# A mixed attention and feed-forward kernel: products nobody reads taken out of round 0, a copy split over two engines, keys and row moves issued in another order

## The chip, the cores and the metric

One core of a Trainium2 chip runs the whole program. The metric is device time in microseconds (us), the median of three runs. TensorE (PE in the profile) multiplies, VectorE (DVE), ScalarE (ACT) and GpSimd (POOL) do the elementwise work, and SyncE (SP) only issues DMAs; ACT issues a few DMAs too. "PEld" is the loading of a matmul's stationary operand.

## The reference, cut to what matters

```python
for t in range(S):                      # attention: B=4, H=8, S=768, D=48
    cur = einsum('bhd,bhe->bhde', u * k_t, v_t)
    y_t = einsum('bhd,bhde->bhe', r_t, state + cur)
    state = w_t[..., None] * state + einsum('bhd,bhe->bhde', k_t, v_t)
x = y as (B*S, H*D)                     # 3072 tokens x 384
x = ((x @ w_a) * (x @ w_b)) @ w_out     # "gated": 1536 wide
h = x @ w_in                            # "leaky": 2048 wide
out = (max(h, 0) + alpha * min(h, 0)) @ w_out2
```

## The kernel before, in words

The attention is worked in eight rounds ("duos", n = 0 to 7). A round takes four pairs of heads over half a sequence, in two streams j = 0 and 1, and has eleven phases. Phase 0 multiplies the leaf blocks (`leaf`). Phases 2 to 6 are the levels 1 to 5 (`level`): a level multiplies keys by queries, stream 0 first and then stream 1, 96 TensorE instructions in all; then DVE scales the keys of stream 0 (`step_k`, L889), merges the first half of the products into `a_sb` (`merge_level`, L905), scales the keys of stream 1 and merges the second half, while the queries are scaled by `step_r` (in round 0 on POOL, L464). The next level's stream j needs the scaled keys and queries of stream j. The last level is not merged but copied into `a_sb` by ACT (`copy_last_level`, four copies of 32 x 384). Phase 7 turns the keys (`turn_keys`, L691), phases 8 and 9 form key-value products (`key_values`, L705) from which DVE carries the states (`carry_states`, L926, one chain a stream), then come `weighted_values` (L719) and in phase 10 `outputs` (L732). ACT copies the outputs out of PSUM (`copy_outputs`), DVE subtracts to get their low parts (`lower_outputs`, L962), and six small DMAs (`move_rows`, L336) move the rows of the last unit from `f_y` into `x_parts`.

The outputs of round n are tile n of the gated layer. Its twelve blocks (`up_a`, `up_b`, `down`, L163 to L165: three products of high and low parts) form the loop over g; one phase of the next round stands between two blocks. Before that loop, steps 0 to 11 (round 0 and the leaf of round 1) run with nothing between them but `keep_clock`: five products of 128 x 384 into `acc[0]` after each of the steps 2 to 8, ten after step 10, and three smaller ones (`keep_clock_early`) about the leaf. Nobody reads them; `acc[0]` is started anew by the first `down`. Before `up_a(0)`, TensorE waits for the copied and lowered outputs and for all six moves (`moved`).

Weights come in pieces of two blocks. SP loads piece p into one of three stages (`load_piece`, six DMAs for a piece of w_a or w_b, one for w_out), ACT splits off the high part (`split_hi`, L135), POOL for the pieces 0 to 5 and DVE after that the low part (`split_lo`, L140), which frees the stage for piece p + 3. `HI_AT` and `LO_AT` give the steps at which ACT and POOL split the pieces 0 to 5; at the steps of `LO_AT` SP also issues the load of piece p + 3. Each engine's queue is in program order, so SP at step 9 stands ahead of SP at step 10, where the moves and then the loads of the next decays (`load_w`) are.

The keys of the next round are scaled by u into `k_scratch` (`prepare_k`) before that round's leaf. In round 0 ACT does this for round 1 at the end of step 10, behind the copying of the outputs and the two moves that it issues itself.

Of the kernel before, what the change touches and what calls it, by code (L numbers as in the profile page):

```python
# [35 lines left out]
HI_AT = [2, 3, 4, 11, 11, 11]  # L36
LO_AT = [7, 8, 9, 11, 11, 11]
X_LOAD, X_SPLIT = 4, 8
OUTPUTS, MOVES = 6, 6
CLOCK_PRODUCTS = 10  # L40
# [145 lines left out]
def copies(duo, what, j, side):  # L186

    return (6 + OUTPUTS) * duo + (0 if what == "level" else 2 + 2 * j) + side + 1


def outputs_copied(duo, part):

    return (6 + OUTPUTS) * duo + 6 + part + 1
# [43 lines left out]
def front(nc, ctx, r, k, w, v, constants, y, alpha, out, shared):  # L237

    with ExitStack() as room, ExitStack() as names:
# [30 lines left out]
        with ExitStack() as room:  # L270
# [17 lines left out]
            products_done, merged, copied = sems("products_done"), sem("merged"), sem("copied")  # L288
            states_done, lowered, moved = sems("states_done"), sem("lowered"), sem("moved")
# [56 lines left out]
            def _(sp):  # L346
# [36 lines left out]
                def move_last_unit(n):  # L383

                    sp.wait_ge(copied, outputs_copied(n, OUTPUTS - 1))
                    sp.wait_ge(lowered, outputs_lowered(n, OUTPUTS - 1))
                    for q in range(KT if n > 0 else 2):
                        for row0 in (0, 64):
                            move_rows(sp, n, q, row0)
# [106 lines left out]
            def _(act):  # L496
# [29 lines left out]
                def copy_last_level(n, hd):  # L526

                    for j in range(2):
                        act.wait_ge(products_done[j], after(n, 5))
                    act.wait_ge(merged, merges(n, 4, 1))  # L530
                    for row0 in (0, 64):
                        done = copy(view(a_sb, S * hd + 32, [[BLOCK, 2 * CH], [1, 32]], 32, row0),
                                    view(products, level_bank(5, hd), [[32, 2 * CH], [1, 32]], 32, row0))
                    done.then_inc(copied, 1)
# [15 lines left out]
                def attend(step):  # L550
                    n, phase = divmod(step, PHASES)
                    if phase == 6:
                        copy_last_level(n, 0)
                    elif phase == 7:
                        copy_kt(n, 0)
                        copy_kt(n, 1)
                    elif phase == 10:
                        copy_outputs(n)
                        if n == 0:
                            act.wait_ge(lowered, OUTPUTS)  # L560
                            for row0 in (0, 64):
                                move_rows(act, n, 2, row0)

                def attend_late(step):
                    n, phase = divmod(step, PHASES)
                    if phase == 6:
                        copy_last_level(n, 1)
                    elif phase == 7 and n + 1 < DUOS:
                        prepare_r(n + 1, 0)
                        if n == 0:  # L570
                            prepare_r(n + 1, 1)
                    elif phase == 8 and 0 < n and n + 1 < DUOS:
                        prepare_k(n + 1, 0)
                        prepare_r(n + 1, 1)
                    elif phase == 9 and 0 < n and n + 1 < DUOS:
                        prepare_k(n + 1, 1)
                    elif phase == 10 and n == 0:
                        prepare_k(n + 1, 0)
                        prepare_k(n + 1, 1)
# [60 lines left out]
            def _(pe):  # L640
# [40 lines left out]
                def turn_keys(n, j):  # L681

                    if j == 0:
                        pe.wait_ge(merged, merges(n, 4, 1))
                    else:
                        pe.wait_ge(copied, copies(n, "level", 0, 1))
# [23 lines left out]
                def weighted_values(n, j):  # L710

                    pe.wait_ge(merged, merges(n, 4, 1))
                    pe.wait_ge(copied, copies(n, "level", 0, 1))
# [103 lines left out]
                def keep_clock(count):  # L817

                    pe.wait_ge(shared.w_hi_ready, 1)
                    w_hi, _ = shared.parts("w_a", 0, 0)  # L820
                    x, _ = shared.parts("w_a", 0, 0, TT)
                    for _ in range(count):
                        pe.matmul(acc[0][:, 0:TT], w_hi, x, start=True, stop=True)  # L823

                def keep_clock_early():

                    pe.matmul(acc[0][:, 0:BANK // 2], k_scratch[0][0:D, 0:P], k_scratch[0][0:D, 0:BANK // 2], start=True, stop=True)

                pe.wait_ge(products_cleared, 1)
                leaf(0, 0)  # L830
                keep_clock_early()
                keep_clock_early()
                leaf(0, 1)
                keep_clock_early()
                for step in range(1, BEFORE_TILES):
                    attend(step)
                    if 2 <= step <= 8:
                        keep_clock(CLOCK_PRODUCTS // 2)
                    elif step == PHASES - 1:
                        keep_clock(CLOCK_PRODUCTS)  # L840
# [18 lines left out]
            def _(dve):  # L859
# [39 lines left out]
                def merge_level(n, hd, phase):  # L899
# [7 lines left out]
                                        view(products, level_bank(phase, hd), [[32, 2 * CH], [h, 32 // h], [1, h]], P)).then_inc(merged, 1)  # L907

# [62 lines left out]
                def attend(step):  # L971
# [20 lines left out]
                    elif phase == 6 and n > 0:  # L992
                        last_step_k(n, 1)
# [288 lines left out]
```

## Time and profile before

| | |
|---|---|
| median of 3 runs | 1037.98 us (1037.82 to 1039.22) |
| the profiled execution's own time | 1041.41 us |
| its span, first to last instruction | 1039.5 us |
| mean granted clock | 0.997 |
| TensorE busy | 1016.9 us (98%) |
| DVE, ACT, POOL busy | 553.0, 295.7, 33.2 us |

All times of rows count from the start of the span. In a row of the timeline, "x96" means 96 instructions merged; the time is that of the whole group, and square brackets give the idle time ahead of it with what ended it. The granted clock is in parts of full speed: 1.00 is 2.4 GHz, 0.50 is 1.2 GHz.

### The profile page before, as it was taken

What the parts mean: (1) busy time and instruction counts of PE and PEld (TensorE: products, weight loads), DVE (VectorE), ACT (ScalarE), POOL (GpSimd) and SP (SyncE); (2) the same over time, 40 slices, a digit from 0 to 9 for tenths busy, and PEclk for the clock granted to TensorE, in tenths of its full rate; (3) what the DMA queues carried; (4) which work ended last, traced back from release to release, by engine and by line L of the source; (5) the groups of instructions that cost most, each with busy time, mean ns of one, the idle gap of its engine ahead of it and who ended that gap; (6) DMA issues with size and microseconds to landing.
All of it is one profiled execution on the core that took longest, in us unless ns stands there. A gap on an engine that the chain in (4) does not pass through costs nothing.

```text
span 1039.5 us, 29138 instructions
## 1 busy us (share of the span) xinstructions
PE 1016.9 (98%) x12499; PEld 988.2 (95%) x12499; DVE 553.0 (53%) x1154; ACT 295.7 (28%) x620; POOL 33.2 (3%) x29
## 2 busy tenths in 40 slices
PE   6879999999999999999999999999999999999998
PEld 5779989999999999999999999999999999999998
DVE  6357664574655645646532345645554555455454
ACT  3243513324224133142222333322222222222211
POOL 3420020000000000000000000000000000000000
PEclk9989999999999999999999999999999999999999
DMA  7244241211301312111011232110101010101000
GB/s 181 75 102 129 75 135 30 58 56 29 90 25 34 84 52 62 29 52 37 3 32 51 72 97 81 42 46 1 46 2 46 1 45 0 45 0 46 1 24 23
DMA packets 42168, 53.03 MB, mean 51 GB/s; under 512 B 5184, under 2 KB 42048, under 8 KB 42048
## 3 DMA queue, kind: packets, MB, share of 16 engines
q1 hardware_dynamic: 40624, 51.04, 17.1%
q8 instruction: 95, 1.56, 0.6%
q10 hardware_dynamic: 1424, 0.23, 0.2%
q14 instruction: 25, 0.20, 0.1%
HBM read 39.46 MB, written 9.44 MB: 47 GB/s over the span
## 4 chain that ended last, share of the span: by engine, by line
PE 94%; DVE 2%; issue 1%; DMA 1%; ACT 1%; SPq 0%; POOL 0%; ACTq 0%; DVEq 0%
PE products L163 17%; PE products L164 16%; PE products L165 16%; PE acc L163 11%; PE acc L165 11%; PE acc L164 11%; PE products L677 6%; PE products L691 1%; PE acc L823 1%; PE products L719 1%; PE products L705 1%; PE products L732 1%; PE products L654 1%; DVE f_y L877 1%; DMA w_v<-in_w_dram 1%
## 5 line engine op out<-in xcount | busy, mean ns | idle before, releaser
L163 PE MATMUL products<-x_parts,weights_hi 128*128 128x384 f32 x576 | 201.8, 350 | 0.9
L164 PE MATMUL products<-x_parts,weights_hi 128*128 128x384 f32 x576 | 195.0, 339 | 0.0
L165 PE MATMUL products<-x_parts,weights_lo 128*128 128x384 f32 x576 | 194.6, 338 | 0.0
L1169 DVE TENSOR_SCALAR leaky_low<-products,leaky_al 128x384 f32<-128x384 f32 x128 | 79.1, 618 | 169.4 <-PE products L165 169.3
L1029 DVE TENSOR_TENSOR g_sb<-a_g,products 128x384 f32<-128x384 f32 x96 | 53.2, 554 | 202.2 <-issue 118.7
L1116 ACT ACTIVATE leaky_g_hi<-leaky_g_sb 128x384 fp32r<-128x384 f32 x128 | 67.3, 525 | 295.0 <-DVE leaky_g_sb L1174 295.0
L498 ACT ACTIVATE g_hi<-g_sb 128x384 fp32r<-128x384 f32 x96 | 50.3, 524 | 244.5 <-DVE g_sb L1029 244.5
L163 PEld LDWEIGHTS products<-x_parts,weights_hi 128*128 128x128 f32 x576 | 108.7, 189 | 5.0 <-issue 1.6
L165 PEld LDWEIGHTS products<-x_parts,weights_lo 128*128 128x128 f32 x576 | 108.9, 189 | 0.0
L164 PEld LDWEIGHTS products<-x_parts,weights_hi 128*128 128x128 f32 x576 | 108.9, 189 | 0.0
L163 PE MATMUL acc<-g_hi,weights_hi 128*128 128x384 f32 x288 | 97.7, 339 | 2.4 <-DVE g_lo L1035 1.8
L165 PE MATMUL acc<-g_hi,weights_lo 128*128 128x384 f32 x288 | 97.5, 338 | 0.0
L164 PE MATMUL acc<-g_lo,weights_hi 128*128 128x384 f32 x288 | 96.9, 336 | 0.0
L498 ACT ACTIVATE a_g<-products 128x384 f32<-128x384 f32 x96 | 47.3, 493 | 132.0 <-PE products L165 132.0
L1035 DVE TENSOR_TENSOR g_lo<-g_sb,g_hi 128x384 fp32r<-128x384 f32 x96 | 53.5, 557 | 38.2 <-ACT g_hi L498 38.0
L1156 DVE TENSOR_TENSOR leaky_g_lo<-leaky_g_sb,leaky_g_hi 128x384 fp32r<-128x384 f32 x128 | 70.4, 550 | 5.2 <-ACT leaky_g_hi L1116 4.7
L677 PEld LDWEIGHTS products<-r_in,k_in 48*64 48x64 f32 (+1 forms) x3840 | 60.7, 139 | 12.4 <-issue 10.5
L1174 DVE SCALAR_TENSOR_TENSOR leaky_g_sb<-products,leaky_low 128x384 f32<-128x384 f32 x128 | 70.6, 552 | 0.3
L677 PE MATMUL products<-r_in,k_in 48*64 48x32 f32 (+1 forms) x3840 | 65.4, 223 | 1.0 <-POOL r_in L464 0.7
L164 PE MATMUL products<-x_parts,leaky_rest_hi 128*128 128x384 f32 x192 | 65.0, 339 | 0.0
L163 PE MATMUL products<-x_parts,leaky_rest_hi 128*128 128x384 f32 x192 | 64.9, 338 | 0.0
L165 PE MATMUL products<-x_parts,leaky_rest_lo 128*128 128x384 f32 x192 | 64.9, 338 | 0.0
(86 smaller groups left out, 1789.4 us busy)
## 6 DMA issues: line engine op xcount, KB each, us to landing
k_in<-in_k_dram SPq DMA_DIRECT2D x16, 336.0 KB, 4.0
r_in<-in_r_dram SPq DMA_DIRECT2D x16, 336.0 KB, 5.2
stage<-in_w_out_dram SPq DMA_DIRECT2D x14, 384.0 KB, 3.2
w_v<-in_v_dram SPq DMA_DIRECT2D x16, 288.0 KB, 3.3
y_dram<-x_in SPq DMA_DIRECT2D x8, 576.0 KB, 3.2
x_in<-y_dram SPq DMA_DIRECT2D x8, 576.0 KB, 4.5
out_dram<-leaky_out_sb SPq DMA_DIRECT2D x7, 576.0 KB, 3.3
stage<-in_w_dram SPq DMA_DIRECT2D x10, 336.0 KB, 4.0
```

Source lines behind the costliest of these rows:

```text
L163: pe.matmul(out, w_hi, x_hi, start=first, stop=False)
L164: pe.matmul(out, w_hi, x_lo, start=False, stop=False)
L165: return pe.matmul(out, w_lo, x_hi, start=False, stop=last)
L498: return act.activation(out, in_, ACT.Copy)
L654: last = pe.matmul(view(products, stream_bank(j, hd) + BLOCK * c, [[1, BLOCK]], BLOCK, BLOCK * par), key_blocks(k_scratch[j], hd, c, par), ...
L677: last = pe.matmul(view(products, level_bank(phase, hd) + 32 * (CH * j + c), [[1, 32]], rows, BLOCK * par), key_blocks(k_in[j], hd, c, par ...
L1029: dve.tensor_tensor(g_sb[:, :], a_g[:, :], b_ps(g), ALU.mult).then_inc(g_ready, 1)
L1035: dve.tensor_tensor(g_lo[f % 2][:, :], g_sb[:, :], g_hi[f % 2][:, :].bitcast(F32), ALU.subtract).then_inc(g_lo_ready, 1)
L1116: return act.activation(out_, in_, ACT.Copy)
L1156: dve.tensor_tensor(self.g_lo[f % 4][:, :], self.g_sb[f % 2][:, :], self.g_hi[f % 4][:, :].bitcast(F32), ALU.subtract).then_inc(self.g_lo_ ...
L1169: dve.tensor_scalar(self.low[f % 2][:, :], h, 0.0, self.al[:, f:f + 1], ALU.min, ALU.mult).then_inc(self.low_ready, 1)
L1174: dve.scalar_tensor_tensor(self.g_sb[f % 2][:, :], h, 0.0, self.low[f % 2][:, :], ALU.max, ALU.add).then_inc(self.g_ready, 1)
```

## The change

It has five parts. (1) All of `keep_clock` and `keep_clock_early` goes, 48 calls. (2) Of the last level's four copies, DVE takes two; ACT's two wait for the merge of their own half only, and `turn_keys` and `weighted_values` wait for both engines. (3) In round 0, ACT prepares the keys of round 1 at step 9, ahead of the outputs. (4) Piece 3 is split at step 9 and not at step 11, high and low part; with it SP loads piece 6 at step 9, ahead of the moves. (5) The moves go block by block: SP moves block 2 as soon as the outputs' parts 0 to 3 are there, and then the others; in round 0, SP moves the blocks 2 and 0 and ACT block 1 (before: SP 0 and 1, ACT 2).

```diff
--- before.py
+++ after.py
@@ -33,11 +33,10 @@
 DUOS, PHASES = UNITS // 2, 11
 F_AT = {2: 0, 4: S // 2, 8: S // 2 + S // 4, 16: S - S // 8, 32: S - S // 16, 64: S - S // 32}
 BEFORE_TILES = PHASES + 1
-HI_AT = [2, 3, 4, 11, 11, 11]
-LO_AT = [7, 8, 9, 11, 11, 11]
+HI_AT = [2, 3, 4, 9, 11, 11]
+LO_AT = [7, 8, 9, 9, 11, 11]
 X_LOAD, X_SPLIT = 4, 8
 OUTPUTS, MOVES = 6, 6
-CLOCK_PRODUCTS = 10
 STAGES = 3
 STAGED_FROM = 3
 
@@ -185,12 +184,12 @@
 
 def copies(duo, what, j, side):
 
-    return (6 + OUTPUTS) * duo + (0 if what == "level" else 2 + 2 * j) + side + 1
+    return (5 + OUTPUTS) * duo + (0 if what == "level" else 1 + 2 * j) + side + 1
 
 
 def outputs_copied(duo, part):
 
-    return (6 + OUTPUTS) * duo + 6 + part + 1
+    return (5 + OUTPUTS) * duo + 5 + part + 1
 
 
 def outputs_lowered(duo, part):
@@ -286,6 +285,7 @@
             f_done, r_stepped = sem("f_done"), sems("r_stepped")
             k_first, k_stepped, k_last = sems("k_first"), sems("k_stepped"), sems("k_last")
             products_done, merged, copied = sems("products_done"), sem("merged"), sem("copied")
+            last_level_copied = sem("last_level_copied")
             states_done, lowered, moved = sems("states_done"), sem("lowered"), sem("moved")
             a_done, b_done, a_copied, g_ready = sem("a_done"), sem("b_done"), sem("a_copied"), sem("g_ready")
             g_hi_ready, g_lo_ready, down_done, x2_copied = sem("g_hi_ready"), sem("g_lo_ready"), sem("down_done"), sem("x2_copied")
@@ -382,9 +382,10 @@
 
                 def move_last_unit(n):
 
-                    sp.wait_ge(copied, outputs_copied(n, OUTPUTS - 1))
-                    sp.wait_ge(lowered, outputs_lowered(n, OUTPUTS - 1))
-                    for q in range(KT if n > 0 else 2):
+                    for q in ((2, 0, 1) if n > 0 else (2, 0)):
+                        part = 3 if q == 2 else OUTPUTS - 1
+                        sp.wait_ge(copied, outputs_copied(n, part))
+                        sp.wait_ge(lowered, outputs_lowered(n, part))
                         for row0 in (0, 64):
                             move_rows(sp, n, q, row0)
 
@@ -523,14 +524,14 @@
                     copy(every_other(r_leaf[j], 1), every_other(queries_of(n, j), 1))
                     scaled(r_leaf[j], queries_of(n, j), 0, j).then_inc(r_prepared[j], 1)
 
-                def copy_last_level(n, hd):
+                def copy_last_level(n):
 
                     for j in range(2):
                         act.wait_ge(products_done[j], after(n, 5))
-                    act.wait_ge(merged, merges(n, 4, 1))
+                    act.wait_ge(merged, merges(n, 4, 0))
                     for row0 in (0, 64):
-                        done = copy(view(a_sb, S * hd + 32, [[BLOCK, 2 * CH], [1, 32]], 32, row0),
-                                    view(products, level_bank(5, hd), [[32, 2 * CH], [1, 32]], 32, row0))
+                        done = copy(view(a_sb, 32, [[BLOCK, 2 * CH], [1, 32]], 32, row0),
+                                    view(products, level_bank(5, 0), [[32, 2 * CH], [1, 32]], 32, row0))
                     done.then_inc(copied, 1)
 
                 def copy_kt(n, j):
@@ -550,7 +551,7 @@
                 def attend(step):
                     n, phase = divmod(step, PHASES)
                     if phase == 6:
-                        copy_last_level(n, 0)
+                        copy_last_level(n)
                     elif phase == 7:
                         copy_kt(n, 0)
                         copy_kt(n, 1)
@@ -559,13 +560,11 @@
                         if n == 0:
                             act.wait_ge(lowered, OUTPUTS)
                             for row0 in (0, 64):
-                                move_rows(act, n, 2, row0)
+                                move_rows(act, n, 1, row0)
 
                 def attend_late(step):
                     n, phase = divmod(step, PHASES)
-                    if phase == 6:
-                        copy_last_level(n, 1)
-                    elif phase == 7 and n + 1 < DUOS:
+                    if phase == 7 and n + 1 < DUOS:
                         prepare_r(n + 1, 0)
                         if n == 0:
                             prepare_r(n + 1, 1)
@@ -574,7 +573,7 @@
                         prepare_r(n + 1, 1)
                     elif phase == 9 and 0 < n and n + 1 < DUOS:
                         prepare_k(n + 1, 1)
-                    elif phase == 10 and n == 0:
+                    elif phase == 9 and n == 0:
                         prepare_k(n + 1, 0)
                         prepare_k(n + 1, 1)
 
@@ -683,7 +682,8 @@
                     if j == 0:
                         pe.wait_ge(merged, merges(n, 4, 1))
                     else:
-                        pe.wait_ge(copied, copies(n, "level", 0, 1))
+                        pe.wait_ge(copied, copies(n, "level", 0, 0))
+                        pe.wait_ge(last_level_copied, n + 1)
                     pe.wait_ge(k_last[j], n + 1)
                     for c in range(CH):
                         for hd in range(2):
@@ -710,7 +710,8 @@
                 def weighted_values(n, j):
 
                     pe.wait_ge(merged, merges(n, 4, 1))
-                    pe.wait_ge(copied, copies(n, "level", 0, 1))
+                    pe.wait_ge(copied, copies(n, "level", 0, 0))
+                    pe.wait_ge(last_level_copied, n + 1)
                     pe.wait_ge(states_done[j], states_after(n))
                     for c in range(CH):
                         for par in range(2):
@@ -814,30 +815,9 @@
                                                  f == 0, f == F1 - 1)
                     product.then_inc(down_done, 1)
 
-                def keep_clock(count):
-
-                    pe.wait_ge(shared.w_hi_ready, 1)
-                    w_hi, _ = shared.parts("w_a", 0, 0)
-                    x, _ = shared.parts("w_a", 0, 0, TT)
-                    for _ in range(count):
-                        pe.matmul(acc[0][:, 0:TT], w_hi, x, start=True, stop=True)
-
-                def keep_clock_early():
-
-                    pe.matmul(acc[0][:, 0:BANK // 2], k_scratch[0][0:D, 0:P], k_scratch[0][0:D, 0:BANK // 2], start=True, stop=True)
-
                 pe.wait_ge(products_cleared, 1)
-                leaf(0, 0)
-                keep_clock_early()
-                keep_clock_early()
-                leaf(0, 1)
-                keep_clock_early()
-                for step in range(1, BEFORE_TILES):
+                for step in range(BEFORE_TILES):
                     attend(step)
-                    if 2 <= step <= 8:
-                        keep_clock(CLOCK_PRODUCTS // 2)
-                    elif step == PHASES - 1:
-                        keep_clock(CLOCK_PRODUCTS)
                 for g in range(TILES * F1):
                     up_a(g)
                     if slot_at(g - 1):
@@ -905,6 +885,16 @@
                     dve.copy_predicated(view(a_sb, S * hd + h, [[BLOCK, 2 * CH], [2 * h, 32 // h], [1, h]], P),
                                         view(level_mask, 32 * (phase - 1), [[0, 2 * CH], [h, 32 // h], [1, h]], P).bitcast(I32),
                                         view(products, level_bank(phase, hd), [[32, 2 * CH], [h, 32 // h], [1, h]], P)).then_inc(merged, 1)
+
+                def copy_last_level(n):
+
+                    for j in range(2):
+                        dve.wait_ge(products_done[j], after(n, 5))
+                    dve.wait_ge(merged, merges(n, 4, 1))
+                    for row0 in (0, 64):
+                        done = dve.tensor_copy(view(a_sb, S + 32, [[BLOCK, 2 * CH], [1, 32]], 32, row0),
+                                               view(products, level_bank(5, 1), [[32, 2 * CH], [1, 32]], 32, row0))
+                    done.then_inc(last_level_copied, 1)
 
                 def carry_states(n, j):
 
@@ -989,8 +979,10 @@
                         if n > 0:
                             step_r(n, 0, phase - 1)
                             step_r(n, 1, phase - 1)
-                    elif phase == 6 and n > 0:
-                        last_step_k(n, 1)
+                    elif phase == 6:
+                        if n > 0:
+                            last_step_k(n, 1)
+                        copy_last_level(n)
                     elif phase == 7 and n > 0:
                         step_r(n, 0, 5)
                         step_r(n, 1, 5)
```

## Rows read from the trace of the kernel before

**Rows 1.** Waits of TensorE over the span: us in total, times, longest.

```profile
PE products L654 <- ACT k_scratch L503: 3.8, 1, 3.8
...
PE acc L163 <- DVE g_lo L1035: 1.8, 1, 1.8
```

**Rows 2.** Timeline of TensorE up to the first tile: start, us, what.

```profile
14.22 2.79 PE L677 MATMUL products<-r_in,k_in 48*64 48x32 f32 x96 [0.29 <-DVE a_sb L895]
...
26.16 1.97 PE L823 MATMUL acc<-weights_hi 128*128 128x384 f32 x5
...
32.67 1.51 PE L677 MATMUL products<-r_in,k_in 48*32 48x32 f32 x96
...
36.00 2.81 PE L691 MATMUL products<-ident,k_in 48*64 48x48 f32 x96
...
40.64 1.21 PE L705 MATMUL products<-w_v,k_scratch 64*48 64x48 f32 x48
...
43.68 0.83 PE L705 MATMUL products<-w_v,k_scratch 64*48 64x48 f32 x48
...
51.12 0.32 PE L732 MATMUL products<-r_in,state 48*48 48x64 f32 x4 [2.06 <-issue]
51.36 2.03 PE L823 MATMUL acc<-weights_hi 128*128 128x384 f32 x10
57.16 2.71 PE L654 MATMUL products<-r_leaf,k_scratch 48*64 48x64 f32 x96 [3.77 <-ACT k_scratch L503]
59.80 0.69 PE L163 MATMUL products<-x_parts,weights_hi 128*128 128x384 f32 x1
```

**Rows 3.** Windows of TensorE: busy, granted clock (PEclk), DMA share, GB/s.

```profile
26.20:28.10 1.90, 1.90 (x13) 1.00 0.00 0
...
59.80:64.10 4.30, 4.30 (x17) 0.50 0.47 132
64.10:70.00 5.90, 5.90 (x35) 0.98 0.58 160
```

**Rows 4.** Timeline of VectorE: level 3, the carried states, the first g_sb.

```profile
26.30 0.58 DVE L905 COPY_PREDICATED a_sb<-level_mask,products 128x384 f32<-128x384 int32 x1 [0.62 <-PE products L677]
26.78 0.94 DVE L889 TENSOR_TENSOR k_in<-k_in,f_y 112x384 f32<-112x384 f32 x1
...
42.22 1.97 DVE L926 SCALAR_TENSOR_TENSOR state<-state,f_y,products 112x48 f32<-112x48 f32 x10
...
65.38 0.56 DVE L1029 TENSOR_TENSOR g_sb<-a_g,products 128x384 f32<-128x384 f32 x1 [4.39 <-issue]
```

**Rows 5.** Timeline of GpSimd, level 3 and the pieces 0 to 2.

```profile
25.15 2.15 POOL L464 TENSOR_TENSOR r_in<-r_in,f_y 112x384 f32<-112x384 f32 x2 [2.42 <-PE products L677]
...
36.92 5.40 POOL L140 TENSOR_TENSOR weights_lo<-stage,weights_hi 128x768 fp32r<-128x768 f32 x3
```

**Rows 6.** Timeline of ScalarE: the last copies, its two moves, piece 6.

```profile
34.29 1.97 ACT L498 ACTIVATE a_sb<-products 32x384 f32<-32x384 f32 x4 [17.39 <-PE products L677]
...
54.17 1.39 ACTq L336 DMA_DIRECT2D x_parts<-f_y  x2
...
66.29 0.85 ACT L135 ACTIVATE weights_hi<-stage 128x768 fp32r<-128x768 f32 x1 [2.72 <-DMA stage<-in_w_a_dram]
```

**Rows 7.** Timeline of SyncE's queue: pieces 3 and 6, the moves.

```profile
39.23 3.99 SPq L130 DMA_DIRECT2D stage<-in_w_a_dram  x6
...
54.21 2.90 SPq L336 DMA_DIRECT2D x_parts<-f_y  x4
...
60.72 4.02 SPq L130 DMA_DIRECT2D stage<-in_w_a_dram  x6
```

**Rows 8.** DMA issues of two stretches: KB each, median us to landing.

```profile
k_in<-in_k_dram SPq DMA_DIRECT2D x1, 336.0 KB, 5.6
...
stage<-in_w_a_dram SPq DMA_DIRECT2D x4, 48.0 KB, 3.6
...
x_parts<-f_y SPq DMA_DIRECT2D x4, 48.0 KB, 2.6
```

## The prediction

> **What bounds the kernel now.** I began with the busy shares in the table above: TensorE is busy for 98% of the span and VectorE for about half, so only time in which TensorE idles, or does work that nobody needs, can be won. The list of TensorE's waits and its timeline show three places to note, all ahead of 76 us: 3.8 us ahead of round 1's leaf, 2.1 us inside the outputs of round 0, and 1.8 us ahead of the second `down` [rows 1, 2]. The timeline of TensorE then gives the plan: from `up_a(0)` at 59.80 us on it is dense to the end, so what the change is worth is how much earlier that instruction starts, and what becomes of the 1.8 us. Everything below follows round 0 engine by engine up to that start.
>
> **The unread products.** Groups of five stand behind the levels 1 to 5, `turn_keys` and the first `key_values`. Between the starts of level 1 (14.22) and level 5 (32.67) lie four periods, so one is 18.45 / 4 = 4.61 us: 2.72 for the 96 level instructions and 1.90 for the five products [rows 2]. Not all of the 1.90 comes back, since the products cover DVE. The chain that is left for a level: the stream 1 half of the level takes half of 2.72, 1.36; its last instruction ends 0.3 later and the merge starts 0.06 after that; DVE merges (0.48 to the start of the next instruction) and scales the keys of stream 1 (0.9), upon which the next level's stream 1 half may start [rows 4]. Together 1.36 + 0.3 + 0.06 + 0.48 + 0.9 = 3.1 us. POOL's two query steps take 2.15 us a level and fit in [rows 5]. Level 1's stream 1 half starts at 14.22 + 1.36 = 15.6 as before (what gates it is the leaf's merge, which the small early products do not cover). Level 2's starts at 18.8 (its merge has POOL and DMA beside it; I give it 0.1 more), then 21.9, 25.0 and 28.1. Level 5 is half as long, so its products are done at 28.1 + 0.7 + 0.3 = 29.1. Before, it was done at 32.67 + 1.51 = 34.2 [rows 2]. The first part therefore gives 5.1 of the 7.6 us that four groups take.
>
> **The shared copy.** ACT's four copies took 1.97 us from 34.29 [rows 6]. With two on each engine, each takes half: 29.1 to 30.1. For DVE's no row exists; a merge of 128 x 384 starts its successor after 0.48 [rows 4], the ACT copy after 0.49, so two are bounded by about 0.5 and 1.2 us (the slower rate of a scaling beside POOL), and I take 1.0. The second half of `turn_keys` starts at 30.2 and is done at 31.9; before, 36.00 + 2.81 = 38.8 [rows 2]. Gain so far 6.9 us: the group behind level 5 adds 1.9, of which the copies eat a little. In later rounds the DVE copies fall into a phase in which DVE has time to spare and TensorE is dense; I cost them at nothing. If that cover were missing, seven rounds of 1.0 us would cost 7 us.
>
> **TensorE's own chain to the outputs.** `key_values` of stream 0 is done at 33.1; ACT's copy lets stream 1 follow, done at 34.2. DVE carries the states: 2.3 us a stream (0.3 ahead of the ten steps of 1.97 [rows 4]), so 35.4 and 37.7. Weighted values to 39.2, then 80 output instructions. At 28 ns each, the rate of the low clock (2.71 us for 96 in the leaf at 57.16 [rows 2, 3]), they take 2.3: done at 41.8. From outputs done (51.45) to lowered and the moves' issue (54.17) before took 2.7 [rows 2, 6], so the outputs are lowered at 44.5. Round 1's leaf need not wait for `prepare_k` any more: the keys' load, issued behind `turn_keys` at 31.9, lands within 5.6 us [rows 8], so both streams are prepared by about 39. The leaf runs from 44.5 to 47.2 and the wait of 3.8 us [rows 1] vanishes. That is not yet `up_a(0)`: it waits for the moves.
>
> **SP's queue, the new bound.** What is added here is piece 6 ahead of the moves. Its load waits for piece 3's low part. POOL's four steps about level 5 ran before from its first half, 33.7, to 36.92 [rows 2, 5], some 0.8 each, and two of them follow its end: 29.1 + 1.7 = 30.8, 6.1 us earlier than 36.92; piece 0 is split at 32.6 (5.40 / 3 is 1.8 each [rows 5]). SP then issues piece 3: 3.99 us, to 36.6 [rows 7]. Its last DMA starts 0.4 before that and lands 2.2 to 3.8 later (the 48 KB ones there took 3.6 [rows 8]); I take 39.2. ACT's high part takes 0.85 [rows 6], POOL's low part 1.84: 42.0. Only now SP issues the six DMAs of piece 6, 4.02 us [rows 7], to 46.0. Behind them stand the four moves, which had been ready at about 44.5: 2.90 us of issue [rows 7], the last begun at 48.3, landed 2.6 later [rows 8]: 50.9. ACT's two moves run beside this and end earlier, and the early block 2 finds SP busy, so part 5 of the change gives nothing in round 0. In later rounds the moves end ahead of their tile already, as TensorE has no wait there [rows 1]. Queued behind the moves, `load_w` for round 1 ends near 50.1 and lands by 55.5; DVE needs it some 8 us after `up_a(0)`, at 58.9.
>
> So `up_a(0)` starts at 50.9 in place of 59.80: 8.9 us.
>
> **After the start.** The first 4.3 us of the tile ran at 0.50, the next stretch at 0.98 [rows 3]; I take the same. Before, ACT split piece 6 at 66.29 once its DMA had landed, with the first g_hi behind it, at 67.05; g_sb had been ready at 65.38 + 0.56 = 65.94 [rows 4]. With piece 6 loaded earlier that pair shifts 1.0 us forward, and with it the DVE chain (keys, queries, decays of round 1) at whose end TensorE waited 1.8 us [rows 1, 6]. Gain 1.0; bounds 0 and 1.8.
>
> **The sum.** 8.9 + 1.0 = 9.9 us. The profiled execution's own 1041.41 (span 1039.5) becomes 1031.5; the median of the runs lies 3.4 below that execution, and 1037.98 - 9.9 = 1028.1.
>
> **The clock, read in two ways.** The ten products at 51.36 take 2.03 us and the five of every earlier group 1.97 [rows 2]: the earlier ones ran at half the rate, the low of the two levels (1.2 and 2.4 GHz), although the granted clock column shows 1.00 there [rows 3], where it seems to hold no record yet. The rate changed between the two `key_values`: 48 took 1.21 and then 0.83 us [rows 2]. So thirty busy microseconds with the products in them ran low. The low rate is in the sum above for the outputs; what the products did buy, some 1.5 us between 43.7 and 51.4, lies in the slack of 46.0 - 44.5 that SP's queue leaves. The Trainium skill (TensorE: Matmul & The Clock Gate, "Why this matters for your kernels") advises to keep TensorE busy and without gaps, since it falls to half rate otherwise. By that rule the products should have held the high clock in round 0, and taking them out should cost half rate into the tile; this trace agrees with it only from 43.7 us on. By the page's reading the result is the fourth rival below, by the rows the sum stands.
>
> **The stall inside the outputs.** 2.06 us between the 76th and the last four instructions [rows 2], where the program has no wait. If it is a matter of instructions not yet delivered, it moves with the count of instructions: some 90 fewer stand ahead of it, so that it would fall into round 1's leaf, where 3.7 us of slack covers it. If it stays where it is, the outputs are lowered at 46.6 and SP waits 0.6. The Trainium skill (Runtime: NRT & Kernel Launch, "Instruction fetch mechanics") says such refills are mostly hidden; by the page the sum has 0 here, by the row at most 0.6.
>
> **The rivals.**
> 1. Forecast: the moves queue behind piece 6. 1028.1, own range 1026.5 to 1029.8. Chance 0.48.
> 2. SP is not the bound: piece 3 lands early and piece 6 issues faster, so that the moves start when the outputs are lowered, 44.5. Then `up_a(0)` starts at 44.5 + 2.3 + 2.6 = 49.4 and the gain is 10.4 plus up to 1.8: 1025.8 to 1027.6. For it: the issue is paced by one long DMA. Chance 0.15.
> 3. The levels keep more of their period. If DVE and POOL slow one another throughout as in level 1's merge, a level takes 3.6, level 5 ends 2 us later and everything follows; with a late piece 3 another 1. Gain 7: 1031. Against it: the rows of level 3 already have both engines at work. Chance 0.16.
> 4. The clock: `up_a(0)` now follows an idle stretch of 3.7 us and not the leaf directly. From the leaf's start to the rise at 64.1 before were 7 us; if the tile's first 7 us run low in place of 4.3, that costs 1.35; if 12, 3.9. 1029.5 to 1032. Chance 0.16.
> 5. The other side: without full-size products in round 0 the clock stays low deep into tile 0. Each microsecond at 0.50 costs 0.5; it decides from 20 us more of it on, at up to 5 slots of the tile; one whole first tile (70 us) low would give 1028 + 35 = 1063. Against it: the tile's own products raised the clock after 4.3 us. Chance 0.03.
> 6. The products hide a wait that ends no earlier, such as DVE's or a DMA's, and `up_a(0)` stays near 59: 1037.5. Against it: nothing that `up_a(0)` waits for has its own clock; all of it hangs on round 0. Chance 0.02.
>
> **The numbers.** Cases 1 and 2 lie between 1025.8 and 1029.8 and hold 0.63; cases 3 and 4 reach to 1032 and beyond with 0.32, of which about half lies under 1031. With 0.3 below and up to 1031.8 above, 1025.5 to 1031.8 holds the time 8 times in 10 and leaves out the far ends of 3 and 4 and the last two cases. Within 0.2% (2 us, about what runs of this kernel can tell from no change) is case 6, slower is case 5, so faster has 0.95.
>
> **What would show it.** In the profile after: levels starting about 3.1 us apart; level 5 done at 29; the ACT and DVE copies side by side; piece 6's DMAs in SP's queue directly ahead of the moves, and the moves later than the lowered outputs; a wait of TensorE for a DMA ahead of `up_a(0)`, near 51; a shorter wait ahead of the second `down`. Wrong would be: moves issued as soon as the outputs are lowered, more than 5 us of low clock behind `up_a(0)`, or new waits of TensorE in the later rounds.

## The result, and the profile after

The changed kernel takes 1032.94 us, median of 4 runs (1031.68 to 1033.17), against 1038.60 us for the kernel before, run beside it (4 runs, 1037.82 to 1039.95). The ratio is 0.994, 95% interval 0.9928 to 0.9952, which lies wholly below 1: the changed kernel is faster, by 5.7 us. Forecast were 1028.1 us and a range up to 1031.8; the time lies 1.1 us above its upper end. The sign was right, and the size of the gain was 0.57 of the 9.9 us forecast.

The profiled execution took 1033.08 us, its span is 1030.9 us. So the two profiled executions differ by 1041.41 - 1033.08 = 8.3 us, the medians by only 5.7. That gap is the question of this study.

The timeline of TensorE in the changed kernel, up to the first tile; these lines answer to [rows 2] (before, level 1 began at 14.22, the last level at 32.67, the keys were turned at 36.00, and the first block stood at 59.80):

```profile
14.71 2.79 PE L676 MATMUL products<-r_in,k_in 48*64 48x32 f32 x96 [1.74 <-DVE a_sb L875]
...
29.77 0.86 PE L676 MATMUL products<-r_in,k_in 48*32 48x32 f32 x48 [0.80 <-DVE k_in L869]
30.57 3.02 PE L691 MATMUL products<-ident,k_in 48*64 48x48 f32 x96
...
40.49 2.35 PE L733 MATMUL products<-r_in,state 48*48 48x64 f32 x80
45.66 2.71 PE L653 MATMUL products<-r_leaf,k_scratch 48*64 48x64 f32 x96 [2.82 <-issue]
51.48 0.66 PE L162 MATMUL products<-x_parts,weights_hi 128*128 128x384 f32 x1 [3.11 <-issue]
```

The reader is to see that the products are gone and the levels lie close; that the 80 output instructions run in one piece, without the idle 2.06 us of [rows 2]; and that between the leaf of round 1 (45.66) and the first block (51.48) TensorE idles for 3.1 us. "issue" here is the wait for the moves (the program has no other wait there that ends so late). The queue of SyncE says why; these lines answer to [rows 7]:

```profile
34.51 2.65 SPq L129 DMA_DIRECT2D stage<-in_w_a_dram  x6
...
43.30 2.65 SPq L129 DMA_DIRECT2D stage<-in_w_a_dram  x6
46.05 3.64 SPq L336 DMA_DIRECT2D x_parts<-f_y  x4
49.74 1.11 SPq L349 DMA_DIRECT2D w_v<-in_w_dram  x2
```

Piece 6 is issued from 43.30 to 45.95, the four moves right behind it; VectorE had lowered the last outputs by 45.56. On ScalarE and VectorE, the shared copy and the early keys, answering to [rows 4, 6]:

```profile
28.70 0.92 DVE L869 TENSOR_TENSOR k_in<-k_in,f_y 112x384 f32<-112x384 f32 x1
...
30.75 1.11 DVE L895 COPY a_sb<-products 32x384 f32<-32x384 f32 x2 [0.63 <-PE products L676]
...
57.06 0.55 DVE L1021 TENSOR_TENSOR g_sb<-a_g,products 128x384 f32<-128x384 f32 x1 [7.60 <-issue]
```

```profile
30.74 0.97 ACT L499 ACTIVATE a_sb<-products 32x384 f32<-32x384 f32 x2 [13.62 <-PE products L676]
...
40.54 0.84 ACT L134 ACTIVATE weights_hi<-stage 128x768 fp32r<-128x768 f32 x1 [1.58 <-DMA stage<-in_w_a_dram]
...
45.59 1.38 ACTq L336 DMA_DIRECT2D x_parts<-f_y  x2
```

The granted clock in windows of TensorE about the first block, answering to [rows 3]:

```profile
45.60:51.40 5.80, 2.71 (x96) 0.52 0.46 98
51.40:55.90 4.50, 4.42 (x14) 0.50 1.05 257
55.90:60.00 4.10, 4.10 (x25) 0.98 0.22 66
```

The tile still begins at the low clock, for 4.5 us. The list of TensorE's waits, answering to [rows 1], has the longest wait for `g_lo` at 0.8 us and not 1.8, but a second one of 0.4 beside it, a new one for `g_sb`, and one for `x_in` that was 0.6 before:

```profile
PE products L162 <- issue: 3.1, 1, 3.1
...
PE acc L162 <- DVE g_lo L1027: 1.2, 2, 0.8
...
PE acc L162 <- ACT x_in L499: 0.8, 1, 0.8
...
PE products L162 <- DVE g_sb L1021: 0.5, 1, 0.5
```

### The profile page after: what moved, and what is told of

It is laid out like the page before. It is cut to its first block, busy times and chain, and to the rows that moved or that the text cites. A ratio compares the mean times of both kernels' runs of the same rounds, so it can differ in the third digit from the quotient of the medians.

```text
span 1030.9 us, 29060 instructions
## 1 busy us (share of the span) xinstructions
PE 1003.5 (97%) x12448; PEld 978.7 (95%) x12448; DVE 561.0 (54%) x1170; ACT 288.1 (28%) x604; POOL 32.8 (3%) x29
## 4 chain that ended last, share of the span: by engine, by line
PE 94%; DVE 2%; issue 2%; DMA 1%; ACT 1%; SPq 0%; DVEq 0%; ACTq 0%
PE products L162 17%; PE products L163 16%; PE products L164 16%; PE acc L162 11%; PE acc L164 11%; PE acc L163 11%; PE products L676 6%; PE products L720 1%; PE products L691 1%; PE products L653 1%; PE products L733 1%; PE products L705 1%; DMA w_v<-in_w_dram 1%; DVE f_y L851 0%; DVE state L916 0%
```

## The experiments

Two theories were put down ahead of the first runs. T1: round 0 of the kernel before costs in most executions what its profile shows, and 3 us are lost elsewhere. T2: that profile shows an execution in which the clock rose late, which the products prevent in most others. All times are medians; ratios are against the kernel before on the same chip, with 95% intervals.

**The kernel before, three times more.** No edit.

> The kernel before, unchanged, timed against itself. It shows the spread of one kernel and gives a second profile of it. T1: the second profile has the same round 0, level 1 to level 5 in 18.4 us and the products of five at 1.97 us. T2: in the second profile some of the groups take 1.0 us and not 1.97, the levels lie closer, and the first block of the tile starts at 56 to 58 us, with the span 2 to 3 us shorter.

> A third profile of the kernel before. The second had the clock risen by 33.8 us and the first block of the tile at 56.1, the first had it risen at 43.7 and the block at 59.8. Theory now (T2): the moment of the rise in round 0 varies from execution to execution, so this one shows a rise at some time between 30 and 50 us, and its span follows: some 0.4 us shorter for each microsecond of earlier rise. Rival: the second profile was the exception, and this one repeats the first within 1 us.

> A fourth profile of the kernel before. So far the clock rose at 43.7, 33.8 and 34.6 us, with the tile's first block at 59.8, 56.1 and 55.9. T2 holds that the first block goes with the rise: within 1 us of 55.9 plus 0.4 us for each microsecond that the rise is later than 34.6. Rival: the block moves without the clock's rise.

Measured: 1038.72 us (12 runs, 1035.63 to 1041.45), 1038.72 (8 runs) and 1038.41 us (8 runs), ratios 0.9997, 1.0006 and 1.0006, each interval around 1. The spread of one kernel is thus 6 us, as wide as the effect studied. In the first profile of this kernel even the last group of five, ahead of the second `key_values`, ran slowly; the timeline of TensorE:

```profile
41.79 1.97 PE L823 MATMUL acc<-weights_hi 128*128 128x384 f32 x5
```

The second profile of it (execution of 1036.86 us, span 1035.1), the same view:

```profile
30.53 1.97 PE L823 MATMUL acc<-weights_hi 128*128 128x384 f32 x5
...
33.79 1.14 PE L823 MATMUL acc<-weights_hi 128*128 128x384 f32 x5
...
38.70 1.15 PE L823 MATMUL acc<-weights_hi 128*128 128x384 f32 x5
...
44.34 2.40 PE L732 MATMUL products<-r_in,state 48*48 48x64 f32 x76
...
56.11 0.69 PE L163 MATMUL products<-x_parts,weights_hi 128*128 128x384 f32 x1
```

The third (1036.70 us, span 1034.9) and the fourth (1037.33 us, span 1035.5), the groups of five behind the last level:

```profile
34.03 1.58 PE L823 MATMUL acc<-weights_hi 128*128 128x384 f32 x5
...
37.08 1.16 PE L823 MATMUL acc<-weights_hi 128*128 128x384 f32 x5
...
55.87 0.69 PE L163 MATMUL products<-x_parts,weights_hi 128*128 128x384 f32 x1
```

```profile
33.90 1.97 PE L823 MATMUL acc<-weights_hi 128*128 128x384 f32 x5
...
37.43 1.14 PE L823 MATMUL acc<-weights_hi 128*128 128x384 f32 x5
...
56.48 0.69 PE L163 MATMUL products<-x_parts,weights_hi 128*128 128x384 f32 x1
```

Five products take 1.97 us at the low level of the clock and 1.14 to 1.16 at the high one. The group behind the last level took 1.14 in the second profile (the clock had risen by 33.8), 1.58 in the third (it rose within the group), 1.97 in the fourth (it rose at about 35.9); in the first, on which the prediction rests, the group at 41.79 was at 1.97 still. The first block goes with it: 56.11, 55.87 and 56.48 in place of 59.80, and the spans of 1035.1, 1034.9 and 1035.5 in place of 1039.5. The fourth fits the expectation (55.9 + 0.4 x 1.3 = 56.4). The late rise has the late block, as T2 has it, and the three early ones lie within 0.6 us of each other. In the second profile the clock also fell again at 44: 76 output instructions took 2.40 us (1.34 at the high level), and its block stands 0.2 us behind the third's although its clock rose sooner. Over the 89 executions of the kernel before that were timed beside the first profiled one the median is 1038.55 us, with a standard deviation of 1.6; 14 of them took more than 1040.9, as the first profiled one did. Over the ten of the changed kernel, below, it is 1032.48 with 0.6.

**The products alone.** The kernel before, with every call of `keep_clock` and `keep_clock_early` out:

```diff
-                leaf(0, 0)
-                keep_clock_early()
-                keep_clock_early()
-                leaf(0, 1)
-                keep_clock_early()
-                for step in range(1, BEFORE_TILES):
+                for step in range(BEFORE_TILES):
                     attend(step)
-                    if 2 <= step <= 8:
-                        keep_clock(CLOCK_PRODUCTS // 2)
-                    elif step == PHASES - 1:
-                        keep_clock(CLOCK_PRODUCTS)
```

> The kernel before with all the unread products taken out and nothing else. Two theories for why the profiled executions differ by 8.3 us (1041.41 to 1033.08) and the medians by only 5.7. T1: round 0 costs in most executions of before what its profile shows, and the missing 3 us are lost elsewhere. Then this kernel gains what the periods of the levels give, 4.6 less 3.3 us each, about 6 us against before: 1032 to 1033. T2: the profiled execution of before is a slow one, in which the clock stayed low through round 0, while in the others the products raise it earlier and round 0 is 3 us shorter. Then this kernel gains only 2 to 4 us: 1034.5 to 1036.5.

Measured: 1032.43 us (6 runs, 1030.48 to 1033.57), ratio 0.9932 (0.9913 to 0.9952), a gain of 6.7 us. That is the whole gain of the change. The median is in T1's range and not in T2's. T2 had taken the early rise for the usual case. The four profiles of before lie toward both ends of its times (three at 1036.7 to 1037.3, one at 1041.4) and the median of 1038.55 in between; against the early ones this kernel's profile (1033.57 us, the slowest of its six executions) gains 3.1 to 3.8 us, against the late one 7.8, and the median gain lies between. So neither theory held whole: the first profile was a slow execution, but the three early ones are faster than the median too. The timeline of TensorE, its leaf of round 1 and the first block:

```profile
41.56 2.54 PE L732 MATMUL products<-r_in,state 48*48 48x64 f32 x80
49.83 2.84 PE L654 MATMUL products<-r_leaf,k_scratch 48*64 48x64 f32 x96 [5.74 <-ACT k_scratch L503]
```

The leaf waits 5.7 us for the keys, and the first block follows at once, at 52.60.

**The other four parts alone.** The changed kernel with the products put back, at the same places.

> The changed kernel with all the unread products put back, so the other four parts of the change alone. Both theories: the leaf of round 1 no longer waits 3.8 us for its keys, but the first block of the tile then waits for the moves, so 1 us is won there and 1 us by the earlier piece 6: 2 us against before, about 1036.5. Where the sum of this gain and that of the kernel with only the products out is well under 5.7 us, the parts help each other.

Measured: 1036.65 us (12 runs, 1034.53 to 1040.80), ratio 0.9979 (0.9963 to 0.9996): 2.4 us gained, as expected. So the parts do not add: 6.7 and 2.4 us by themselves, 5.4 to 5.7 together. The times spread over 6.3 us here and over 1.5 and 1.7 us in the two timings of the changed kernel, which differs from this one by the products alone.

**The products and the keys.** To the kernel with the products out, only part 3 of the change is added:

```diff
-                    elif phase == 10 and n == 0:
+                    elif phase == 9 and n == 0:
                         prepare_k(n + 1, 0)
```

> The kernel before with all the unread products out and round 1's keys prepared at step 9 in place of step 10, nothing else of the change. Asks why the whole change gains no more than the products alone. Theory: the wait of 5.7 us for the keys ahead of round 1's leaf goes to 2.7, but the first block then waits for the moves, issued from 46.9 to 49.8 and landed by 51.7, in place of 52.6: 0.9 us of the 3 are kept, 1031.5 to 1032. Rival: the moves land early, and all 3 us are kept: 1029.5.

Measured: 1031.53 us (6 runs, 1030.64 to 1031.74), ratio 0.9935 (0.992 to 0.995). The timelines of TensorE and SyncE:

```profile
45.04 2.84 PE L654 MATMUL products<-r_leaf,k_scratch 48*64 48x64 f32 x96 [2.81 <-ACT x_parts L498]
50.40 0.66 PE L163 MATMUL products<-x_parts,weights_hi 128*128 128x384 f32 x1 [2.51 <-issue]
```

```profile
45.02 3.64 SPq L336 DMA_DIRECT2D x_parts<-f_y  x4
48.70 1.10 SPq L349 DMA_DIRECT2D w_v<-in_w_dram  x2
```

The leaf starts as soon as the outputs are lowered, but the first block idles 2.5 us for the moves: what the keys gave is taken by the next wait. With two parts of five this kernel stands where the whole change stands (its span 1028.8 us, 1030.9 and 1029.8 there). The profiles also show what part 2 gives where it was meant to: from the start of `turn_keys` to its end TensorE takes 3.7 us with ACT's four copies (here and with the products out) and 3.0 with the shared ones, 0.7 us less.

**Piece 6 behind the moves.** The changed kernel with

```diff
-HI_AT = [2, 3, 4, 9, 11, 11]
-LO_AT = [7, 8, 9, 9, 11, 11]
+HI_AT = [2, 3, 4, 11, 11, 11]
+LO_AT = [7, 8, 9, 11, 11, 11]
```

> The changed kernel with piece 3 split at step 11 again, so that piece 6 is loaded behind the moves and not ahead of them. Theory of the forecast, SP's queue is the bound ahead of the first block: its profile had the moves begin at 46.05, the outputs lowered at 45.5, so at most 0.6 us is won at the start, and the later piece 6 costs about 1 us behind the first block: 1033 to 1034, no gain. Rival, the piece ahead of the moves costs the whole of its 2.65 us of issue: 1031 or less.

Measured: 1032.19 us (6 runs, 1031.07 to 1033.31), ratio 0.9932 (0.9913 to 0.9952). Not to be told from the changed kernel. The timeline of SyncE:

```profile
45.56 2.71 SPq L336 DMA_DIRECT2D x_parts<-f_y  x4
```

The first block stands at 51.00, 4.6 us behind the last lowering of the outputs (46.42); in the first profile of the changed kernel it stood 5.9 us behind it (45.56 to 51.48). So in these profiles piece 6 ahead of the moves costs 1.3 us, more than the 0.6 expected; the block came only 0.5 us earlier because round 0 itself ran 0.9 us later here. Behind the block 979.6 us were left, against 979.4: no price of the later piece 6 can be read from that. The medians do not show the 1.3 us, and why they do not stays open.

**The changed kernel again.** No edit.

> The changed kernel unchanged. T2: without the products round 0 stays at the low clock in every execution, so its profile repeats within 1 us (first block at 51 to 52 us) and its times spread less than those of before (35.6 to 42.3 there). Ratio to before 0.993 to 0.995. Rival: the changed kernel varies as much, and the ratio's interval holds 0.990.

Measured: 1032.40 us (6 runs, 1031.34 to 1033.03), ratio 0.994 (0.9925 to 0.9955), first block at 50.76. Its times spread over 1.7 us, those of before beside it over 5.2. In its profile the clock rose too, for a moment: the 80 output instructions took 1.53 us, against 2.35 in the first profile, and the leaf behind them 2.84 us, at the low level again. (In the first profile too it had risen by the end of the outputs: the granted clock falls between 45 and 46, where it is 0.93.) SyncE's queue decided what came of it:

```profile
42.72 2.65 SPq L129 DMA_DIRECT2D stage<-in_w_a_dram  x6
45.47 3.50 SPq L336 DMA_DIRECT2D x_parts<-f_y  x4
```

The outputs were lowered at 44.37, 1.2 us sooner than in the first profile, but piece 6 held the moves back to 45.47, and the first block came only 0.7 us sooner.

**The moves shared three and three.** The kernel with piece 6 behind the moves, with ACT taking one move more:

```diff
-                        for row0 in (0, 64):
+                        for row0 in ((0,) if n == 0 and q == 0 else (0, 64)):
                             move_rows(sp, n, q, row0)
...
-                            for row0 in (0, 64):
-                                move_rows(act, n, 1, row0)
+                            for q, row0 in ((0, 64), (1, 0), (1, 64)):
+                                move_rows(act, n, q, row0)
```

> The changed kernel with piece 3 at step 11 (as in the run with piece 6 behind the moves) and with the six moves of round 0 shared 3 and 3 between SP and ACT, SP's first two issued while the last outputs are lowered. Theory: the first block waits for the last move to land, so it starts about 1 us earlier, at 49.7 to 50.3 us, and the kernel gains 0.5 to 1 us: 1031.5. Rival: what ends last is the landing and not the issue, the block stays at 51: 1032.2.

Measured: 1033.49 us (6 runs), ratio 0.995 (0.9934 to 0.9967), first block at 51.32: no gain, rather a loss, though the interval overlaps with that of the kernel it was made from. SyncE, done sooner, turned to the loads of the next decays, and ACT's moves ran beside them: 3.31 us for three of them. The run shows the two side by side, not that the one slows the other.

```profile
44.52 2.07 SPq L336 DMA_DIRECT2D x_parts<-f_y  x3
46.64 2.08 SPq L349 DMA_DIRECT2D w_v<-in_w_dram  x2
```

```profile
45.41 3.31 ACTq L336 DMA_DIRECT2D x_parts<-f_y  x3
```

**Products where TensorE idles anyway.** Here unread products stand only in the two gaps ahead of the first block, in the changed kernel:

```diff
                 for step in range(BEFORE_TILES):
                     attend(step)
+                    if step == PHASES - 1:
+                        keep_clock(7)
+                    elif step == PHASES:
+                        keep_clock(8)
```

> The changed kernel with 7 unread products of 128 x 384 in the idle 2.8 us behind round 0's outputs and 8 in the idle 3.1 us behind round 1's leaf, which the profile shows ahead of the first block. Theory: the clock of the tile's first 4.6 us is low because TensorE idles there; the products cost nothing and raise it sooner, so up to 2.3 us are won: 1030.5 to 1031.5. Rival: the clock rises no sooner for them, and the products delay the block: 1033 to 1034.

Measured: 1031.92 us (6 runs, 1029.79 to 1036.46), ratio 0.9945 (0.9925 to 0.9964). In the profiled execution, the fastest of the six, the clock is up before the first block (0.41 in place of 0.66 us for its first product):

```profile
42.99 2.61 PE L824 MATMUL acc<-weights_hi 128*128 128x384 f32 x7
45.88 2.13 PE L653 MATMUL products<-r_leaf,k_scratch 48*64 48x64 f32 x96 [0.28 <-issue]
47.94 1.66 PE L824 MATMUL acc<-weights_hi 128*128 128x384 f32 x8
50.46 0.41 PE L162 MATMUL products<-x_parts,weights_hi 128*128 128x384 f32 x1 [0.85 <-issue]
```

With 8 and 14 products:

> The changed kernel with 8 and 14 unread products in the two gaps (7 and 8 before, whose profile had the clock up from the first block on and 0.9 us still idle; its profiled execution took 1029.8, the others 1031.7 to 1032.1). Theory: with the second gap filled the clock stays up in every execution, 1030 to 1031. Rival: where the clock is low at that point, 14 products take 4.5 us in place of 2.5 and delay the block, so the executions spread as those of before do: 1031.5 to 1033, some at 1034.

Measured: 1030.67 us (6 runs, 1029.98 to 1033.62), ratio 0.993 (0.9912 to 0.9947), the lowest median of all; its profile has the clock up from the leaf on. With 8 and 8 and piece 6 behind the moves:

> The changed kernel with piece 3 at step 11 again (piece 6 behind the moves) and 8 and 8 unread products in the two gaps. Theory: both gains are small and add, 0.2 from the earlier moves and 0.5 to 2 from the clock: 1030.5 to 1031.5. Rival: piece 6, landed later, sets the first g_hi where the tile now begins at the high clock, and the gain is lost in the wait ahead of the second down: 1032.

Measured: 1031.38 us (6 runs, 1030.15 to 1035.54), ratio 0.9939 (0.992 to 0.9959); its waits for g_lo ahead of `down` came to 2.8 us in place of 1.2, as the rival had it (2.2 us with 7 and 8 products). All three have medians 0.5 to 1.7 us below the changed kernel's 1032.4, and all three have one execution well above the rest (1036.46, 1033.62, 1035.54). Their intervals overlap with that of the change, so none is shown to be faster than it.

## Why the prediction was wrong

**The step that failed** is the last one of the sum: "the median of the runs lies 3.4 below that execution, and 1037.98 - 9.9 = 1028.1". It carried the offset over as if it were the same for both kernels. It is not: the profiled execution of the changed kernel (1033.08) lies 0.1 us above the median of its runs (1032.94). That makes 3.3 of the 4.9 us by which 1028.1 was too low; the other 1.6 are terms of the sum, below. With all executions taken together the first profile of before stands 1041.41 - 1038.55 = 2.9 us above its kernel's median, that of the changed kernel 1033.08 - 1032.48 = 0.6 us above its own; so of the 8.3 us between the profiles 2.3 belong to which execution was profiled.

The offset is, as far as profiles show, the late rise of the clock (43.7 in place of 34 to 36 us, 3.3 to 3.9 us at the first block), and the spread that it comes from hangs on the very products that the change removes: with them back in the changed kernel the times have a standard deviation of 1.8 us (12 executions), without them of 0.6 (10). The text had seen their effect on the clock ("what the products did buy, some 1.5 us between 43.7 and 51.4, lies in the slack") but took one moment of the rise as given. Of the unprofiled executions no trace exists, and their mean granted clock does not tell: 43 of the executions of before have 0.997, and they reach from 1035.6 to 1042.3 us. That their spread has the clock as its cause is therefore argued, not shown. Rival 4 spoke of the clock behind the first block; that was not it: 4.5 us ran low there, against 4.3 before.

**On the scale of the profiles** the sum was 9.9 and 8.3 came. Term by term:
- The start of the first block: 8.9 forecast, 59.80 - 51.48 = 8.3 measured. The path was the forecast one: piece 3, its high part (40.54), its low part (41.46 to 43.27), piece 6, the moves. That the moves began at 46.05, for 46.0 forecast, was luck in part, since two errors cancelled: everything ahead ran late (level 1 by 0.5 us, the second half of the last level at 29.77 for 28.1, piece 3 issued from 34.51 for 32.6), but the pieces 3 and 6 took 2.65 us each to issue and not 3.99 and 4.02. What was missing is in the moves themselves: 3.64 us of issue and not 2.90. The outputs were lowered at 45.56 for 44.5, so the moves waited 0.5 us for the queue, and 1.1 in the second profile, not 1.5.
- Behind the block: 1.0 forecast, 979.7 - 979.4 = 0.3 measured (span less the block's start), and less than that by the other profiles: 979.0 in each of the three others of before, 979.0 in the second of the changed kernel. The longest wait for `g_lo` did go from 1.8 to 0.8, but the second one of 0.4, 0.5 for `g_sb` and 0.2 more for `x_in` took it back.
- Outside the span: 1.9 us before, 2.2 after, a cost that the sum did not have. It is no accident of the profiles: it is 1.7 to 2.0 us in 85 executions of before, and 2.1 to 2.2 in every execution of the changed kernel and of the kernels made from it. With the products alone out, and with the keys early as well, it stays at 1.7 to 1.9, and with piece 3 late it is still 2.1 to 2.2, so it comes with part 2 or part 5. Why stays open.

**Period of the levels.** 3.1 us were forecast from DVE's chain; the second halves of level 1 and of the last level lie 13.7 us apart, 3.4 each. Rival 3 (3.6 us) had this in part. **The shared copy** took 1.11 us on DVE for the 1.0 taken, beside ACT's 0.97. **The stall in the outputs** is gone from there, as taken; in the four profiles of before it took 2.1, 0.6, 1.4 and 1.7 us. In the changed kernel's two profiles TensorE idles 0.8 and 0.5 us behind the 55th of the 96 `key_values` instructions, where the program has no wait either, and not in round 1's leaf, to which the text had let it move. What the stall is, and whether this is the same one, stays open; the Trainium skill (Runtime: NRT & Kernel Launch, "Instruction fetch mechanics") would have such refills mostly hidden, and no run here tells whether it is one. **Later rounds** cost nothing that can be seen, as forecast: behind the block the changed kernel's two profiles have 979.4 and 979.0 us, those of before 979.0 to 979.7.

**The page on the clock.** The Trainium skill (TensorE: Matmul & The Clock Gate, "Why this matters for your kernels") asks for a busy TensorE without gaps. The traces agree in part: the rise in round 0 came in all four profiles of before, yet 20 to 30 us of full occupation stood ahead of it; without the products it came too, in some profiles and late (the outputs at the high rate in two, weighted values in one). What the products cost, 1.9 us a group at the low level, is more than the earlier high clock gave back: 6.7 us net by their removal.

**Left open:** why the rise comes at 33.8 in one execution and 43.7 in another; and which of the parts 2, 4 and 5 gives anything once 1 and 3 are in. Part 2 and part 5 were not tried by themselves, nor was the rest of the change without them.

## What to carry to other kernels

Time the same kernel many times before you trust one profile of it: where a stretch depends on something that varies from run to run (here the moment at which the clock rises), add a term of the sum to the profile's own time only after asking whether the profile's distance from the median belongs to the part that is taken out. Filler work that is to hold a clock up has to be timed against leaving it out: here it cost 6.7 us, and placed only where the engine idles it was not shown to gain either. And when a wait is removed ahead of a start that has several conditions, look up the next one first: here TensorE idled 1.6 to 3.4 us for the moves once the keys were early.

## What the runs showed of the hardware

- In the profiles of before TensorE was occupied without a gap to speak of from 14 us to the rise of the clock, by small instructions (28 ns apart at the low level) with five products of 128 x 384 between them, and the clock was at 1.2 GHz till 33.8, 34.6, 35.9 and 43.7 us. It rose with small instructions alone too, in some profiles: with no product in round 0, 80 output instructions took 1.53 us at 40.12 in one profile of the changed kernel and 2.35 at 40.49 in the other. The granted clock column shows 1.00 for all of this; the durations, 1.97 and 1.14 us for five products, tell the level.
- Three small DMAs of 48 KB issued by ACT took 3.31 us beside two loads of 336 KB from SyncE's queue, against 1.38 us for two in the changed kernel.
- 35 executions of one unchanged kernel on one core of one chip reached from 1035.6 to 1042.3 us.
